# A fused attention, mixture and gated-MLP kernel: score steps of both expert pairs go tile by tile, and the row scales ride in the pad columns of the turned probabilities

## What is computed

```python
kv = einsum('bhsd,bhse->bhde', k, v)
out = einsum('bhsd,bhde->bhse', q, kv)
x = out / sqrt(mean(out * out) + 1e-6) * g_norm          # 576 x 512 per batch
logits = x @ w_gate                                      # 4 experts, the top 2 are taken
w = exp(sel - max(sel)); w /= sum(w) + 1e-9
for e in range(4):
    scores = scale * (x @ wq[e]) @ (x @ wk[e]).T         # causal
    a = exp(scores - max(scores)); a /= sum(a) + 1e-9
    y += mask[e] * w[e] * (a @ (x @ wv[e]) @ wo[e])
h = gelu(y @ w_in); u, v = split(h)
v_n = (v - mean(v)) / sqrt(var(v) + 1e-6) * g_ln
v_s = w_sg @ v_n + b_sg
result = y + (u * v_s) @ w_out
```

## Time and profile before

| | us |
|---|---|
| median of 3 runs (853.58 to 854.58) | 854.56 |
| the profiled execution | 854.5 |
| its span in the trace | 852.6 |
| TensorE matmuls busy | 835.2 (98%) |
| VectorE busy | 461.4 (54%) |
| ScalarE busy | 403.1 (47%) |
| POOL busy | 185.3 (22%) |

### The profile page before, as it was taken

How to read it: one execution, slowest core, us unless ns; L and a number is a source line. 1 busy time by engine, 2 the same in 40 slices (tenths; PEclk the granted TensorE clock), 3 DMA queues, 4 the chain that set the end, 5 groups by cost and what they waited for, 6 DMA issues and landing times.

```text
span 852.6 us, 17275 instructions
## 1 busy us (share of the span) xinstructions
PE 835.2 (98%) x6717; PEld 734.3 (86%) x6717; DVE 461.4 (54%) x1345; ACT 403.1 (47%) x979; POOL 185.3 (22%) x236
## 2 busy tenths in 40 slices
PE   7988999999999999999999999999999999999998
PEld 4787898889888898988989889888988889898796
DVE  1666744475535655477534674447553565537640
ACT  1558613573236732476233761457423673247621
POOL 1402233012410133102230123301232013310220
PEclk9999999999999999999999999999999999999999
DMA  9913314003130034101250031500414000100001
GB/s 277 237 33 102 101 41 107 1 2 112 33 86 1 2 113 80 44 1 49 65 105 13 1 92 37 110 1 2 112 31 88 1 2 2 44 25 2 1 1 62
DMA packets 117408, 47.32 MB, mean 55 GB/s; under 512 B 94352, under 2 KB 110736, under 8 KB 117328
## 3 DMA queue, kind: packets, MB, share of 16 engines
q1 hardware_dynamic: 117328, 46.21, 21.8%
HBM read 35.19 MB, written 9.44 MB: 52 GB/s over the span
## 4 chain that ended last, share of the span: by engine, by line
PE 92%; DVE 4%; ACT 2%; issue 1%; DMA 0%; DVEq 0%; ACTq 0%
PE w L985 36%; PE t L985 23%; PE t L1048 7%; PE t L1032 7%; PE w L1016 6%; PE t L1144 3%; PE t L1130 2%; PE w L1198 2%; PE t L1152 2%; PE w L1102 2%; DVE big L818 1%; ACT probs L638 1%; DVE work L940 1%; PE t L1062 1%; DVE work L948 1%; DVE qT_uT L956 1%
## 5 line engine op out<-in xcount | busy, mean ns | idle before, releaser
L985 PE MATMUL t<-big,wqk_s 128*128 128x288 f32 x768 | 110.2, 298 | 1.7 <-DVE big L892 1.2
L985 PE MATMUL w<-wout_s,big 128*128 128x512 f32 x432 | 108.1, 399 | 1.5 <-DVE big L818 0.5
L985 PE MATMUL w<-wsgT_s,big 128*128 128x288 f32 x768 | 107.6, 296 | 0.0
L985 PEld LDWEIGHTS t<-big,wqk_s 128*128 128x128 f32 x768 | 102.9, 188 | 2.6 <-issue 2.3
L985 PEld LDWEIGHTS w<-wsgT_s,big 128*128 128x128 f32 x768 | 104.1, 189 | 0.0
L638 ACT ACTIVATE probs<-w,neg_max 128x64 f32<-128x64 f32 (+4 forms) x160 | 83.0, 525 | 33.0 <-DVE neg_max L771 30.3
L985 PEld LDWEIGHTS w<-wout_s,big 128*128 128x128 f32 x432 | 79.6, 188 | 20.3 <-DVE big L818 3.2
L542 POOL TENSOR_TENSOR yT<-squares,yT 128x256 fp32r<-128x256 f32 (+1 forms) x32 | 22.3, 698 | 304.6 <-ACT yT L672 304.5
L771 DVE CUSTOM_DVE_ANT_0 w<-w,causal 128x64 f32<-128x64 f32 (+4 forms) x160 | 75.3, 512 | 8.7 <-PE w L1016 7.5
L653 ACT ACTIVATE work<-t 128x384 f32<-128x384 f32 (+3 forms) x160 | 63.3, 454 | 31.2 <-PE t L1032 29.7
L686 ACT ACTIVATE big<-work 128x576 fp32r<-128x576 f32 x32 | 22.0, 686 | 111.9 <-POOL work L561 96.4
(11 more groups left out here) (114 smaller groups left out, 1357.1 us busy)
## 6 DMA issues: line engine op xcount, KB each, us to landing
kin<-in_k_dram SPq DMA_DIRECT2D x8, 1024.0 KB, 6.3
vin<-in_v_dram SPq DMA_DIRECT2D x8, 1024.0 KB, 9.3
out_dram<-work SPq DMA_DIRECT2D x32, 256.0 KB, 2.1
qin<-in_q_dram SPq DMA_DIRECT2D x112, 72.0 KB, 2.4
staged_win<-in_moe_w_in_dram SPq DMA_DIRECT2D x4, 512.0 KB, 5.2
staged<-in_moe_w_sg_dram SPq DMA_DIRECT2D x4, 288.0 KB, 3.9
kin<-in_k_dram SPq DMA_DIRECT2D x8, 128.0 KB, 2.9
vin<-in_v_dram SPq DMA_DIRECT2D x8, 128.0 KB, 7.3
```

The lines of the kernel that those rows point to most:

```text
L985: last = nc.tensor.matmul(o, stationary(hs, c), mv(hm, c), start=c == of[0] and p == 0, stop=c == of[-1] and p == len(PASSES) - 1)
```

## The change

The unit of the score steps becomes a tile with both expert pairs. tile_scores(t) puts the scores and exponentials of steps 2t and 2t + 1 together; ("T", t) turns the 4(t + 1) blocks of both pairs in units of four blocks (eight in the wide slots for tile 4), whose copies ("T_copy", (t, i)) are shared between ScalarE and VectorE (T_DVE); values(t) weights both pairs. probs gets a second buffer in staged, pT a second one in qT_uT, taken by turns. The row scales of a tile are made by one set of three operations, scale_rows(t), whose last writes them over the pad columns of probs, which lie in the first block of each head: the transposes of the probabilities turn them too, and they come out on partitions 0 to 63 of that block. spread_scales, its slot and ScalarE's copy of it are gone. y_scaled multiplies y by them straight out of pT, in one operation for each half of the partitions. The value rows that they meet in the weighting are those of the pad tokens, which are zero; for that POOL now clears the pad columns of qT_uT in every batch (at u, 0). gate_ranks, g_exp and gate_weights become units of their own. Narrow slots are named one by one (SLOT) where the ring stood, except for o and x.

In batch 0 w_sg is staged in vin and qin instead of staged, the last three transposes of it and wsgR come behind y of tile 4, the wout parts go between the u products, the kv product behind the vs products, and SP's loads of q for batch 1 wait until wsgR is done, ahead of the loads of k and v.

```diff
-    T_GROUPS = {t: ([(0, t + 1)] if t < 4 else [(0, 3), (3, 5)]) for t in range(NT)}
...
+    T_UNITS = {t: [4] * (t + 1) if t < NT - 1 else [8, 8, 4] for t in range(NT)}
+    T_SLOT = {0: ["t0"], 1: ["t1", "t2"], 2: ["t3", "t1", "t2"], 3: ["t3", "t1", "t2", "t0"], 4: ["w0", "w1", "t3"]}
+
+    T_DVE = {(1, 0), (2, 0), (2, 2), (3, 1), (3, 3), (4, 0), (4, 2)}
+    Y_SLOT = {0: "t0", 1: "t0", 2: "t3", 3: "t0", 4: "t0"}
...
-    def attention(late_qk, late):
-
-        plan = []
-        for m in QK_ORDER:
-            plan += [("qk", (m, 0))] + late_qk.get(m, [])
-        for n in range(N - 2):
-            plan += [("s", n)] + [("scale", n - 1)] * (n >= 1) + [("t", n - 2)] * (n >= 2)
-            plan += [("spread", n // 2 - 2)] * (n >= 4 and n % 2 == 0) + [("yhi", n // 2 - 2)] * (n >= 5 and n % 2 == 1)
-            plan += [("exp", n)]
-            plan += (late.get(n, []) if n == 0 else []) + BETWEEN.get(n, []) + (late.get(n, []) if n > 0 else [])
-            plan += [("pv", n - 3)] * (n >= 3)
-        return plan + [("t", N - 4), ("spread", NT - 3), ("scale", N - 3), ("s", N - 2), ("exp", N - 2), ("pv", N - 5),
-                       ("t", N - 3), ("yhi", NT - 3), ("spread", NT - 2), ("pv", N - 4), ("s", N - 1), ("scale", N - 2), ("exp", N - 1)]
...
+    def tile_scores(t):
+
+        return [("s", 2 * t), ("s", 2 * t + 1), ("exp", 2 * t), ("exp", 2 * t + 1)]
+
+    def copies(t, *among):
+        return [("T_copy", (t, i)) for i in among]
+
+    def values(t):
+        return [("pv", 2 * t), ("pv", 2 * t + 1), ("y_mul", t), ("yhi", t)]
...
+        plan += [("qk", (0, 1)), ("ranks", 0), ("qk", (EP, 1)), ("g_exp", 0), ("weights", 0), ("scale", 0), ("qk", (1, 1)),
+                 ("scale", 1)] + late(("split", "wo")) + [("qk", (EP + 1, 1)), ("T", 0), ("T", 1)]
+        plan += copies(0, 0) + copies(1, 0, 1) + tile_scores(2) + [("v", 4), ("scale", 2)] + values(0)
+        plan += tile_scores(3) + [("T", 2)] + copies(2, 0, 1, 2) + [("ranks", 1), ("scale", 3)] + values(1)
+        plan += [("s", N - 2), ("T", 3)] + copies(3, 0) + [("exp", N - 2)] + copies(3, 1, 2, 3)
+        return plan + values(2) + [("s", N - 1), ("exp", N - 1)]
...
+    def mlp(first, last):
+        plan = [("h", 0), ("g_exp", 1), ("weights", 1), ("scale", NT - 1), ("h", 1), ("gelu", 0), ("gelu", 1)] + values(3)
+        plan += [("T", 4)] + copies(4, 0, 1, 2) + [("h", 2), ("h", 3), ("pv", N - 2), ("pv", N - 1), ("gelu", 2),
+                 ("y_mul", NT - 1), ("yhi", NT - 1)]
+        if first:
+            plan += [("wsgT", 2), ("wsgT", 3), ("gelu", 3), ("wsgT", 4), ("wsgR", 0)]
+        elif last:
+            plan += [("gelu", 3)]
+        else:
+            plan += [("gelu", 3)] + KV
+        return plan + [("h", 4), ("gelu", 4)]
...
+    MIX_FIRST = [x for m in range(FC) for x in (("u", m), ("wout", m))] + MIX[FC:] + KV
+    PLAN = {-1: FIRST, 0: attention(True) + mlp(True, False) + MIX_FIRST + MIXED_ONE}
...
-                def scale_probs(n):
-
-                    t, e = n // 2, n % 2
-                    for g, (lo, hi) in enumerate(GATES):
-                        if t == lo and e == 0:
-                            gate_weights(g, lo, hi)
-                    for V, _ in score_slots(n):
-                        u.wait_drained(dve, part, V)
-                    nc.vector.tensor_scalar(row_sum[:, n, :], row_sum[:, n, :], 1e-9, None, ALU.add).then_inc(row_step, 1)
-                    dve.wait_ge(row_step, count(part, 2 * N, 2 * n + 1))
-                    nc.vector.reciprocal(row_inv[:, n, :], row_sum[:, n, :]).then_inc(row_step, 1)
-                    dve.wait_ge(row_step, count(part, 2 * N, 2 * n + 2))
-                    if t >= 2 and e == 0:
-                        dve.wait_ge(spread_full, count(part, NT - 1, t - 1))
+                def scale_rows(t):
+
+                    for n in (2 * t, 2 * t + 1):
+                        for V, _ in score_slots(n):
+                            u.wait_drained(dve, part, V)
+                    sums, invs = row_sum[:, 2 * t:2 * t + 2, :], row_inv[:, 2 * t:2 * t + 2, :]
+                    nc.vector.tensor_scalar(sums, sums, 1e-9, None, ALU.add).then_inc(row_step, 1)
+                    dve.wait_ge(row_step, count(part, 2 * NT, 2 * t + 1))
+                    nc.vector.reciprocal(invs, sums).then_inc(row_step, 1)
+                    dve.wait_ge(row_step, count(part, 2 * NT, 2 * t + 2))
                     nc.vector.tensor_tensor(
-                        row_scale[t % 2][:, e, :].rearrange("p (a d) -> p a d", a=2),
-                        row_inv[:, n, :].rearrange("p (a d) -> p a d", d=1).to_broadcast([P, 2, HD]),
-                        gate[:, t, 2 * e:2 * e + 2].rearrange("p (a d) -> p a d", d=1).to_broadcast([P, 2, HD]),
+                        probs[t % 2][:, :, :, 0:PAD].rearrange("p e a n -> p (e a) n"),
+                        invs.rearrange("p e (a d) -> p (e a) d", d=1).to_broadcast([P, E, PAD]),
+                        gate[:, t, :].rearrange("p (f d) -> p f d", d=1).to_broadcast([P, E, PAD]),
                         ALU.mult).then_inc(row_scaled, 1)
 
...
+                def y_scaled(t):
+                    x = src(("y", t))[:, 0:2 * P].rearrange("p (e n) -> p e n", e=EP)
+                    if count(part, NT, t) > 1:
+                        dve.wait_ge(yT_lo, count(part, NT, t - 1))
+                    spread = pT[t % 2][:, 0:P * E * (t + 1)].rearrange("p (e a n) -> p e a n", e=EP, a=2)
+                    for a in range(2):
+                        rows = slice(HD * a, HD * (a + 1))
+                        last = nc.vector.tensor_tensor(y_t[t % 2][rows, :].rearrange("p (e n) -> p e n", e=EP), x[rows, :, :],
+                                                       spread[0:HD, :, a, 0:P], ALU.mult)
+                    give(last, ("y", t))
+
...
-                    elif kind == "pv":
-                        if j % 2 == 1:
-                            t = j // 2
-                            U = ("y", t)
-                            x = src(U)[:, 0:2 * P]
-                            if t < NT - 1:
-                                dve.wait_ge(spread_copied, count(part, NT - 1, t + 1))
-                            else:
-                                u.wait_drained(dve, part, ("spread", t))
-                            if count(part, NT, t) > 0:
-                                dve.wait_ge(yT_lo, count(part, NT, t))
-                            give(nc.vector.tensor_tensor(y_t[:, :], x, scale_t[:, :], ALU.mult), U)
-                            if t == NT - 1:
-                                y_low(t)
...
-                def transpose_probs(n, g):
-                    if g == 0:
-                        for V, _ in score_slots(n):
-                            u.wait_drained(pe, part, V)
-                    lo, hi = T_GROUPS[n // 2][g]
-                    for a in range(2):
-                        V = ("t", n, a, g)
+                def transpose_probs(t):
+
+                    pe.wait_ge(row_scaled, count(part, NT, t + 1))
+                    blocks = [(e, a, b) for e in range(EP) for a in range(2) for b in range(t + 1)]
+                    for i, w in enumerate(T_UNITS[t]):
+                        V = ("T", t, i)
                         x = dst(V)
-                        for b in range(lo, hi):
-                            last = nc.tensor.transpose(x[:, P * (b - lo):P * (b - lo + 1)],
-                                                       probs[:, n % 2, a, P * b:P * (b + 1)], ident[:, :])
+                        for r, (e, a, b) in enumerate(blocks[first_block(t, i):first_block(t, i) + w]):
+                            last = nc.tensor.transpose(x[:, P * r:P * (r + 1)], probs[t % 2][:, e, a, P * b:P * (b + 1)],
+                                                       ident[:, :])
                         finish(last, V)
 
...
-                def spread_scales(t):
-
-                    pe.wait_ge(row_scaled, count(part, N, 2 * t + 2))
-                    V = ("spread", t) if t == NT - 1 else ("y", t)
-                    if t >= NT - 2:
-                        u.wait_free(pe, part, V)
-                    x = ps[u.slot(part, V)]
-                    for e in range(EP):
-                        last = nc.tensor.transpose(x[:, P * (EP + e):P * (EP + e + 1)], row_scale[t % 2][:, e, :],
-                                                   ident[:, :])
-                    if t == NT - 1:
-                        finish(last, V)
-                    else:
-                        last.then_inc(spread_full, 1)
-
                 for kind, j in PLAN[part]:
                     U = (kind, j)
```

214 lines of the change are left out of this document (109 added, 105 removed).

## The result

The changed kernel takes 866.88 us (median of four runs, 863.27 to 867.95) where the kernel before takes 854.50 beside it (four runs, 853.58 to 854.58): a ratio of 1.014, 95% interval 1.011 to 1.017. The forecast was 854.6 with a range of 847 to 861. Run again on another chip beside three of the experiments it gave 867.87 (867.62 to 868.90), a ratio of 1.016 [1.014, 1.018].

What follows compares the result with a forecast made beforehand. TensorE, busy 835.2 of 852.6 us, was taken as the bound: an inner batch is spared 3.9 but gains waits of 0.4 + 2.6 + 0.9; 6 x (+0.14) - 0.6 - 0.1 = +0.1 us gives 854.6, range 847 to 861.

Steps and rivals of the forecast that it cites:

- T1: Turns of tile 1: TensorE waits 0.4 us a batch for VectorE's scales.
- scores of tile 4 and T3 together: TensorE waits 2.6 us a batch: 1.5 before tile 4's scores (tile 3's exponentials hold both slots), the rest before tile 3's turns.
- h(3): Fourth hidden product: TensorE waits 0.9 us a batch for the low part of y(3), made by POOL.
- What TensorE is spared: TensorE's work in an inner batch's stretch falls 3.9 us, from 54.0 to about 50.2, by dropped transposes and fewer changeovers.
- scale pairs: Ten transposes of row scales a batch go; a pair is worth 0.23 us, five pairs 1.1.
- scores, ten groups to six: Each group of score matmuls costs 0.24 us above its columns; four groups fewer a batch save 1.0.
- the -0.6 said: First batch's stretch, with new steps and waits counted: 60.2 us against 60.8, so 0.6 shorter.
- A: Rival, faster: VectorE's chain is shorter than summed, so TensorE waits less; 845 us expected; chance 0.16.
- B: Rival, slower: y_scaled's halves cost more than the kvd copy pair; 862.8 us at twice 0.68; chance 0.15.
- C: Rival, slower: batch 1's k and v land late behind q loads; TensorE waits 2.6 us once, 857; chance 0.05.
- D: Rival: no changeover is saved, spared work is 1.1 us, waits shrink equally; within 2 us of forecast; chance 0.02.
- The last sentence of the prediction: The forecast fails at its first step if TensorE's busy sum falls by much more or less than 31 us.

Runs made afterwards that it cites:

- Late ranks: Changed kernel with the ranks of the second gate group moved behind the last maxima on VectorE: 853.12 us against 854.0 for the kernel before, ratio 0.9987.
- the low part moved forward: Changed kernel, ranks later, tile 3's weighting and multiplication earlier, GpSimd's low part of y(3) ahead of h(1)'s root: 845.32 us against 854.28 for the kernel before.
- taken out alone: Kernel before without the five spread pairs of each batch and ScalarE's copies of them, nothing moved, output wrong: 848.51 us, ratio 0.9923.
- the small forms: Kernel before with small multiplications ahead of two u products a batch: 867.75 us in the whole array's form, 873.23 us in half-array forms.
- one wait of 1.6 a batch: Kernel before with a GpSimd power that TensorE awaits ahead of the scores of tile 4: 867.34 us, ratio 1.0155.
- the kernel before with its two main waits: Kernel before with two GpSimd powers that TensorE awaits, ahead of the scores of tile 4 and of the next group: 876.89 us, ratio 1.028.
- y as one operation: Changed kernel with y_scaled as one multiplication on 128 partitions instead of two on 64, output wrong: 850.62 us, ratio 0.9961 to the kernel before.
- waits of 4.44 and 0.88 between whole-array products: Kernel before with two GpSimd powers that TensorE awaits ahead of the second and third u products: 921.47 us, ratio 1.0786.

## Why the prediction was wrong

**What bounds the kernel, and the waits: right.** Places, engines and sizes came out: T1 0.4 (0.50), scores of tile 4 and T3 together 2.6 (1.62 + 0.92), h(3) 0.9 (0.75). The terms that the prediction lists for h(3) add up to 4.6 and not to its 4.45; with 4.6 it would have said 1.1, further from what came. The prices on VectorE (scale 0.42 at its end, halves 0.85) were measured as taken. Late ranks and the low part moved forward each gave back the whole of their wait, 0.98 and 0.94 a batch.

**What TensorE is spared: the first step that failed.** 3.9 was said, 3.1 measured. By the table of kinds (without what shows of a group's end in front of a wait):

| term | said | measured |
|---|---|---|
| scale pairs | 1.1 | 0.9 (taken out alone) |
| scores, ten groups to six | 1.0 | 0.65 |
| weighting, ten to five | 0.8 | 0.68 |
| turns | 0.5 | 0.4 |
| projections, h, k and v less cut | 0.5 | 0.46 |

The largest error is in the scores. 0.24 was the distance of a group's time from its columns at full rate, and I counted all of it as changeover; a merged group gave back 0.16. The rest of it stays with the matmuls: twelve over 448 columns take 1.43 from start to start, where twice the group of six was 1.60. The pair had the same error: 0.18 for 0.23. With 3.1, an inner batch is 54.0 - 3.1 + 3.8 = 54.7, as measured, and the sum would have been 0.6 x 7 = 4.2 higher, 858.8: slower, and inside the range.

**The clock: the second step that failed, and the one that decided.** "Its granted clock is full throughout" was a reading of a kernel whose TensorE never waited in this stretch, and it was carried over to one that waits 3.3 in each batch. It had no term in the sum. In the profiled execution three falls cost about 5.1 (1.7 and 1.8 by the stretches of the batches 2 and 6, the third about as much). In the repeat at 0.988, the clock of seven executions out of eight, there are six, worth some 9 to 10 of the 13.1 us by which its span is longer than that of before. By the 858.8 above the kernel would have come out within the range but for the falls. Sum for the profiled execution: 4.2 + 5.1, 0.65 for a later start (it varies by 1.7 between executions of these kernels), -0.5 for batch 0 beyond the -0.6 said, -0.7 in the parts behind the stretches: 8.7, and the span is 8.8 longer.

**The rivals.** A (shorter chain) didn't come: the waits were as long as summed. B (dearer halves) didn't: 0.85. C (k and v late) didn't, there is no wait at the kv products of batch 0. D is refuted by the small forms: a change of form costs time. The sign turned out as B had it, for reasons that none of the rivals held. The last sentence of the prediction did its work: TensorE's busy sum fell by 16.4, about 21.5 if the falls are taken out, and not by 31.

**Open.** What decides whether one pair of waits brings a fall and the same pair in the next batch doesn't. The runs show that waits alone can bring it, that it came behind 11 of 32 pairs and behind none of 40 single waits of 1.6 at the same place, and that one wait of 1.6 a batch left three executions of four at 1.000. Between the changed kernel (0.988) and the kernel before with its two main waits (0.998) there remain 0.01 that the wait at T1, the wait at h(3) or the merged order must account for; no run separates these.

## What to carry over

A merged group doesn't give back all that its small groups cost above their columns: price the merge by a merged group from the trace, or take one out. When a change trades TensorE's work against waits, count each wait together with the chance that the clock falls behind it (1.4 to 1.8 us a time here), so an even trade in time was a loss here. And before giving up such a change, look at what stands ahead of the late operation on its own engine: three moves (the ranks later and the multiplication of y(3) earlier for VectorE, the low part ahead of a root on GpSimd) turned 1.4% slower into 1.0% faster.

## What was not expected of the hardware

The granted clock fell from 2.4 to 1.2 GHz behind waits of 1.73 and 0.85 us with a group of scores between (batch 2 of the changed kernel), in a program in which TensorE is busy 95% of the time, and with y as one operation even behind 0.94 and 0.83. A fall lengthens the work behind it by 1.4 to 1.8 us. Behind waits of 4.44 and 0.88 between whole-array products it lasted over two u products (3.22 and 5.85 for 12 and 24 matmuls, where 12 take 1.76) in five batches of eight, and over the first alone in the other three. Even the kernel before shows a lower mean now and then: in each of three sets of its runs one execution had 0.998, at 856.47, 856.59 and 856.63 us, where the medians are 854.0 to 854.5.
